# A chunked recurrence and two dense layers on one core: units of 64 tokens of all batches, and two tensor segments per chunk

## The chip, the cores and the metric

The kernel runs on one core of a Trainium2 chip. The metric is the device time of one execution in microseconds (us). Three executions of the kernel before took 1132.85, 1128.9 and 1137.99 us; the median is 1132.85 us. An "engine" here is TensorE (PE, matmuls), VectorE (DVE), ScalarE (ACT), GpSimd (POOL) or SyncE (SP, which issues most of the transfers).

## The reference

There are 4 batches, 8 heads, 768 tokens and a head size of 40. Each of the 32 sequences (batch, head) carries a 40 by 40 state through its tokens:

```python
for t in range(S):
    y[:, :, t] = np.einsum('bhd,bhde->bhe', rt, state)
    Sa = np.einsum('bhde,bhe->bhd', state, at)
    state_decay = state * wt[:, :, None, :] - np.einsum('bhd,bhe->bhde', Sa, bt)
    state = state_decay + np.einsum('bhd,bhe->bhde', vt, kt)
```

The output, as 3072 tokens by 320 features, goes through two layers. Layer 1 is `h = x @ w_in; x = max(0.01 h, h) @ w_out` with 2048 hidden features. Layer 2 is `sigmoid(x @ w_gate) * (x @ w_val) @ w_out` with 1536 hidden features. All of it is float32.

## The kernel before

**Recurrence.** The 768 tokens are cut into 6 blocks of 128 tokens and each block into 2 halves of 64 tokens. A *unit* u is 128 tokens (block u // 2) of half of the batches, so there are NU = 12 units. A unit has two *chunks* of 64 tokens, n = 2u and 2u + 1, so there are NT = 24 chunks. A chunk holds 16 sequences, as TQ = 8 pairs; the two sequences of a pair lie in partitions 0 to 63 and 64 to 127 (`half(0)`, `half(1)`). The second chunk of a unit needs the state that the first one leaves; the first chunk of a unit needs the state of the second chunk of unit u - 2.

Within a chunk the recurrence is turned into small matmuls. Each function named below issues 8 or 16 pairs of them; the profile records each float32 matmul twice, so 16 small matmuls are "x32":
- `pe_a_ka` (L630, L636) makes the scores of b and k with a, for unit g + 2 and unit g + 1. From the b scores ScalarE makes `p_sb` (`act_a`), SP writes it to DRAM and loads it back in another layout (`store_p`, `load_p_top`, `load_p_low`), and VectorE inverts a triangular matrix column by column (`inverse_columns`, L1252 and L1256, 31 columns per unit, each column waiting for the one before). `store_t` and `load_t` bring the inverse back as `t_sb`.
- `pe_rhs_begin`, `pe_rhs_end` (L658, L662) make the right-hand side from v and from the state. `pe_first` (L698) and `pe_cross` (L708) apply the inverse within the upper 32 tokens and carry it to the lower 32. `pe_ut_u` (L731, L734) makes u in both layouts.
- `pe_sn` (L719) transposes the state. `pe_st` (L748) makes the state's update, which VectorE adds and decays (`dve_st`). `pe_vrur` (L760, L762) makes the scores with r, which VectorE masks (`dve_vrur`, L1285). `pe_y_begin` (L774, state part) and `pe_y_end` (L783) make y. `pe_kb` (L649, L651) transposes k and b.

Between two such functions ScalarE or VectorE empties the PSUM bank. The recurrence uses banks 4 to 7. `claim`, `filled`, `emptied` and `multiplied` are waits on the bank's two counters `bank_filled` and `bank_emptied`.

**Layer 1** works on one block of 512 tokens (128 tokens of 4 batches) at a time, in 16 steps m per block: `up_products` (L808, 8 matmuls of 128x512 into bank 0), `act_g` and `dve_g_low` on the result (float32 values are split into a high part, `g_hi`, and a low part, `g_lo`, L1301), then `down_products` of the step before (L823 to L828, 8 matmuls into banks 1 to 3). Weights and x are split the same way. **Layer 2** follows (`gate_val_products` L858, `down2_products` L876 to L878).

**Order.** Every engine has its program written out in order; each waits for semaphores in that order. Before, the loop goes over windows g (one unit each) of 8 slots s. In each slot PE does one step m = 8g + s - LAG of layer 1 (LAG = 18, so that m = 0 falls in slot 2 of window 2) and one group of the recurrence: at s = 0 `rhs`, `sn`, `first`; at s = 1 `cross`, `a_ka`, `ut_u`; at s = 2 `st`, `vrur`; at s = 3 `rhs` of the second chunk woven with `y_begin` of the first, `y_end`, `first`; at s = 4 `cross`, `a_ka`, `ut_u`, `sn`; at s = 5 `st`, `vrur`; at s = 6 `y_begin`, `y_end`, between the up and the down products; at s = 7 `kb` of both chunks. Before m = 0 there is no layer 1 work; there `fill` (L894) issues matmuls of the identity that nobody reads, as a table says. The last 18 steps of layer 1 run without recurrence.

**Weights of layer 1** come in 8 pieces into a staging tile of 4 places (`load_piece` on POOL's queue); ScalarE writes the high parts (`split_hi`) and VectorE the low parts (`split_lo`) in windows 0 and 1.

## Time and profile before

| what | value |
|---|---|
| runs | 1128.9, 1132.85, 1137.99 us, median 1132.85 |
| profiled execution: its own time | the page gives none beside its span |
| profiled execution: span | 1129.2 us, 36605 instructions |
| first step of layer 1 starts | 158.38 us |
| first `gate_val_products` of layer 2 starts | 733.09 us |
| mean granted TensorE clock | 0.973 |

The profile is of one execution by the hardware profiler. "Busy" is the time in which an engine executed something; a wait is idle time. Small matmuls overlap each other, so the time of a group of them is read from the start of the group to the start of the next one. `PEclk` is the granted TensorE clock as a share of 2.4 GHz: 1.00 is 2.4 GHz and 0.50 is 1.2 GHz. The share of waits marked "issue" is time in which the engine waited for nothing that the profile shows.

### The profile page before, as it was taken

The page shows a single profiled execution, that of the slowest core. Times are in us where ns is not written, and L with a number is a line of the kernel's source. Part 1 is how long each engine was busy: PE and PEld are TensorE (multiplying, and loading weights), DVE is VectorE, ACT ScalarE, POOL GpSimd, SP SyncE. Part 2 cuts the span into 40 slices and gives each one's busy share as a digit, 9 for nine tenths or more (in the row PEclk, how much of TensorE's full clock was granted, in tenths as well). Part 3 has the DMA queues.
Part 4 walks back from the last instruction along what each step waited for, and adds up shares of the span by engine and source line. Part 5 has one row for each costly group of instructions (what it writes and reads, how often), then busy time and mean ns, then how long its engine had stood idle before and what let it go on. Part 6 is the DMA issues. An engine that isn't in the chain of part 4 may idle for free.

```text
span 1129.2 us, 36605 instructions
## 1 busy us (share of the span) xinstructions
PE 1072.3 (95%) x16106; PEld 917.0 (81%) x16106; DVE 595.8 (53%) x1306; ACT 397.3 (35%) x782; POOL 146.4 (13%) x179
## 2 busy tenths in 40 slices
PE   2888979999999999999999999999999999999998
PEld 2777868888888887788788788888888888888887
DVE  7797786767676776667574224443223232323222
ACT  2142243344444443533343335542222222222222
POOL 6313030403122121303010000000000000000000
PEclk9977679999999999999999999999999999999999
DMA  5836363344335342434333024220201002020000
GB/s 176 252 103 151 68 129 80 82 110 123 85 75 134 89 108 62 125 90 100 64 110 79 9 91 145 80 89 1 61 1 57 5 1 61 1 61 1 24 1 23
DMA packets 133856, 87.62 MB, mean 78 GB/s; under 512 B 98274, under 2 KB 113634, under 8 KB 133700
## 3 DMA queue, kind: packets, MB, share of 16 engines
q1 hardware_dynamic: 126740, 62.85, 22.8%
q0 software_dynamic: 6960, 22.45, 6.6%
q8 instruction: 127, 2.08, 0.8%
q14 instruction: 29, 0.24, 0.1%
HBM read 66.39 MB, written 18.87 MB: 76 GB/s over the span
## 4 chain that ended last, share of the span: by engine, by line
PE 89%; issue 4%; DVE 3%; ACT 1%; POOL 1%; DMA 0%; SPq 0%; ACTq 0%; POOLq 0%; DVEq 0%
PE bank L808 16%; PE bank L858 12%; PE pair L858 12%; PE bank L823 4%; PE bank L878 4%; PE bank L876 4%; PE bank L877 4%; PE bank L824 4%; PE bank L825 4%; PE bank L894 3%; PE bank L783 2%; PE bank L760 2%; PE bank L774 2%; PE bank L630 2%; PE bank L828 2%
## 5 line engine op out<-in xcount | busy, mean ns | idle before, releaser
L1301 DVE TENSOR_TENSOR g_lo<-g_full,g_hi 128x512 fp32r<-128x512 f32 x168 | 125.3, 746 | 229.8 <-ACT g_hi L1064 229.6
L1064 ACT CAST g_hi<-g_full 128x512 fp32r<-128x512 f32 x168 | 104.3, 621 | 134.7 <-DVE g_full L1354 131.6
L808 PE MATMUL bank<-x_hi,w_up 128*128 128x512 f32 x480 | 134.7, 410 | 3.6 <-issue 3.6
L1057 ACT ACTIVATE g_full<-bank 128x512 f32<-128x512 f32 x96 | 57.5, 599 | 210.0 <-PE bank L808 204.7
L1256 DVE TENSOR_TENSOR t_unit<-t_unit,prod 128x126 f32<-128x126 f32 (+22 forms) x372 | 106.5, 286 | 12.8
L1252 DVE TENSOR_TENSOR prod<-t_unit,p_unit 128x126 f32<-128x126 f32 (+22 forms) x372 | 102.1, 275 | 20.1 <-DMA p_unit<-p_dram 7.0
L808 PEld LDWEIGHTS bank<-x_hi,w_up 128*128 128x128 f32 x480 | 85.4, 189 | 23.0 <-issue 4.5
L1354 DVE TENSOR_TENSOR g_full<-pair,h_sb 128x512 f32<-128x512 f32 x36 | 24.9, 692 | 112.7 <-PE pair L858 112.0
L808 PE MATMUL bank<-x_lo,w_up 128*128 128x512 f32 x288 | 82.1, 393 | 0.0
L823 PE MATMUL bank<-g_hi,w_dn 128*128 128x512 f32 x192 | 76.4, 398 | 0.4 <-DVE g_lo L1301 0.2
L824 PE MATMUL bank<-g_hi,w_dn 128*128 128x512 f32 x192 | 75.0, 391 | 0.0
L1354 DVE TENSOR_TENSOR g_full<-bank,h_sb 128x512 f32<-128x512 f32 x36 | 24.9, 692 | 94.6 <-PE bank L858 86.3
L825 PE MATMUL bank<-g_lo,w_dn 128*128 128x512 f32 x192 | 74.8, 390 | 0.0
L808 PEld LDWEIGHTS bank<-x_lo,w_up 128*128 128x128 f32 x288 | 54.5, 189 | 12.2
L858 PE MATMUL pair<-x_hi,up 128*128 128x512 f32 x240 | 62.8, 391 | 0.0
L858 PE MATMUL bank<-x_hi,up 128*128 128x512 f32 x240 | 62.8, 391 | 0.0
L878 PE MATMUL bank<-dn,g_lo 128*128 128x320 f32 x192 | 59.3, 309 | 0.0
L877 PE MATMUL bank<-dn,g_hi 128*128 128x320 f32 x192 | 59.3, 309 | 0.0
L876 PE MATMUL bank<-dn,g_hi 128*128 128x320 f32 x192 | 59.1, 308 | 0.0
L630 PE MATMUL bank<-a_sb,b_sb 40*64 40x64 f32 x768 | 33.6, 248 | 23.0 <-POOL a_sb L301 21.6
L630 PEld LDWEIGHTS bank<-a_sb,b_sb 40*64 40x64 f32 x768 | 29.9, 159 | 25.7 <-issue 23.1
L858 PEld LDWEIGHTS bank<-x_hi,up 128*128 128x128 f32 x240 | 44.1, 188 | 7.9
(146 smaller groups left out, 2401.0 us busy)
## 6 DMA issues: line engine op xcount, KB each, us to landing
p_unit<-p_dram SPq DMA_DIRECT2D x48, 128.0 KB, 2.9
stage<-in_w_out POOLq DMA_DIRECT2D x7, 640.0 KB, 5.8
v_tok<-in_vT SPq DMA_DIRECT2D x12, 320.0 KB, 3.1
v_nu<-in_vN SPq DMA_DIRECT2D x24, 160.0 KB, 5.9
x<-y_sb SPq DMA_DIRECT2D x48, 80.0 KB
k_sb<-in_kF POOLq DMA_DIRECT2D x22, 160.0 KB, 3.4
v_sb<-in_vF SPq DMA_DIRECT2D x22, 160.0 KB
r_sb<-in_rF SPq DMA_DIRECT2D x22, 160.0 KB
```

Of the source, the lines that this page charges most:

```text
L808: last = nc.tensor.matmul(up_bank(m)[:], lhs, rhs, start=(e == 0), stop=(e == len(products) - 1))
L823: nc.tensor.matmul(bank[1 + kk][:], w_high, hi, start=(f == 0), stop=False)
L824: nc.tensor.matmul(bank[1 + kk][:], w_low, hi, start=False, stop=False)
L825: nc.tensor.matmul(bank[1 + kk][:], w_high, lo, start=False, stop=(f == NF1 - 1))
L858: last = nc.tensor.matmul(o[:], lhs, rhs, start=(x == 0), stop=(x == len(products) - 1))
L876: nc.tensor.matmul(o, g_hi[:, par, tok], wt[:, 0, f % GT], start=(f == 0), stop=False)
L877: nc.tensor.matmul(o, g_hi[:, par, tok], wt[:, 1, f % GT], start=False, stop=False)
L878: last = nc.tensor.matmul(o, g_lo[:, par, tok], wt[:, 0, f % GT], start=False, stop=(f == NF2 - 1))
L1064: nc.scalar.copy(g_hi[:, m % 2], g_full[:]).then_inc(g_hi_ready, 1)
L1252: nc.vector.tensor_tensor(terms, t_unit[:, 0:m, t:t + 1].to_broadcast([P, m, rest]), p_unit[:, t, t + 1:C].unsqueeze(1).to_broadcast([P, m ...
L1256: nc.vector.tensor_tensor(t_unit[:, 0:m, t + 1:C], t_unit[:, 0:m, t + 1:C], terms, ALU.add).then_inc(column_ready, 1)
L1301: nc.vector.tensor_tensor(g_lo[:, m % 2], g_full[:], g_hi[:, m % 2].bitcast(F32), ALU.subtract).then_inc(g_lo_ready, 1)
```

## The change

- **Units.** A unit is now 64 tokens of all batches; its two chunks are the two halves of the batches. Chunk n needs the state of chunk n - 2, no longer of chunk n - 1. The host lays the inputs out accordingly. Chunks 0 and 1 have no state, so their state matmuls are left out, and so are the state updates of the last two chunks.
- **Order.** The loop goes over chunks n with 4 slots each, m = 4n + s - 22. The recurrence has two segments per chunk: at s = 1 `rhs_begin(n)`, `sn(n-1)`, `vrur(n-1)`, `rhs_end(n)`, `st(n-1)`, `first(n)`; at s = 3 `cross(n)`, the scores (`a` of n + 4, `ka` of n + 1, woven with the state part of y of n - 1), `y_end(n-1)`, `ut_u(n)`, `kb(n+1)`. `fill` is gone.
- **Banks.** `st` and `y` go to bank 0, which they share with the up products; `ut` and `u` share banks 4 and 5; `sn` lies beside `rhs` in the same two banks.
- **Halves.** In every odd pair q the two sequences change places between partitions 0 to 63 and 64 to 127 in part of the operands (`side(i, q)`), also in v and r, which the host swaps.
- **Loads.** b, k, r and v are loaded per chunk instead of per unit; r and v have one place each instead of two. The vrur products have their own tile `vru`; the layer 1 output is evicted into `x_f`.
- **Weights.** Each layer 1 piece is loaded into its own final place and split there, with `x_f` as a scratch place for 64 rows; there is no staging tile. The splits move from before layer 1 to chunks 4 to 7, two pieces per chunk, at s = 2 and 3.

```diff
-LAG = 18
+LAG = 22
+        BANKS = dict(rhs=(4, 5), vrur=(6, 7), st=(0,), first=(6,), a=(6,), ka=(7,), y=(0,), utu=(4, 5), kb=(6, 7))
+        SLOT_X = [("rhs", 0), ("vrur", -1), ("st", -1), ("first", 0)]
+        SLOT_Y = [("a", 4), ("ka", 1), ("y", -1), ("utu", 0), ("kb", 1)]
...
@@ gpsimd_program
+            for n in range(-4, NT):
+                if n >= 0:
+                    fetch_k(pool, n + 2)
+                    fetch_b(pool, n + 4)
+                if chunk(n + 4):
+                    pool_a(pool, n + 4)
+                    pool_b(pool, n + 4)
+                if chunk(n + 2):
+                    pool_k(pool, n + 2)
+                if n >= 0:
+                    fetch_a(pool, n + 5)
+                if n == -1:
+                    pool.wait_ge(p_low_loaded, 32)
+                    load_piece(pool, 0)
+                    load_piece(pool, 1)
...
@@ sync_program
+            for n in range(NT + 2):
+                if n >= 2:
+                    store_y(sp, n - 2)
+                    load_v(sp, n - 1)
+                    load_r(sp, n - 1)
+                if n % 4 == 1 and n >= 5:
+                    load_x(sp, (n - 5) // 4)
+                if n >= 1:
+                    store_p(sp, n + 3)
+                if n % 2 == 0 and n >= 2:
+                    load_p_top(sp, (n + 2) // 2)
+                    load_p_low(sp, (n + 2) // 2)
+                load_w(sp, n + 5)
+                if n % 2 == 0 and n >= 2:
+                    load_v_nu(sp, n // 2)
+                if n % 2 == 1:
+                    load_v_tok(sp, (n + 1) // 2)
+                    store_t(sp, (n + 1) // 2)
+                    load_t(sp, (n + 1) // 2)
...
+        def side(i, q):
+            return i if q % 2 == 0 else 1 - i
...
@@ up_products
             wait(pe, g_ready, m if m <= DENSE else m - 1)
+            wait(pe, bank_emptied[0], turns_before_up[m])
...
-        FILL = {("kb", -1): 2, ("sn", 0): 56,
...
@@ tensor_program
+                    if s == 1:
+                        if chunk(n):
+                            pe_rhs_begin(pe, n)
+                        if has_state(n - 1):
+                            pe_sn(pe, n - 1)
+                        if chunk(n - 1):
+                            pe_vrur(pe, n - 1)
+                        if chunk(n):
+                            pe_rhs_end(pe, n)
+                        if has("st", n - 1):
+                            pe_st(pe, n - 1)
+                        if chunk(n):
+                            pe_first(pe, n)
+                    elif s == 3:
+                        if chunk(n):
+                            pe_cross(pe, n)
+                        pe_scores(pe, n + 4, n + 1, n - 1)
+                        if chunk(n - 1):
+                            pe_y_end(pe, n - 1)
+                        if chunk(n):
+                            pe_ut_u(pe, n)
+                        if chunk(n + 1):
+                            pe_kb(pe, n + 1)
...
@@ vector_program
                     if s == 1:
+                        if n % 4 == 1 and 5 <= n < 4 * NJ + 5:
+                            dve_x(dve, (n - 5) // 4)
+                        if chunk(n - 1):
+                            dve_vrur(dve, n - 1)
+                        if has("st", n - 1):
+                            dve_st(dve, n - 1)
+                    elif s == 3:
...
+                            if chunk(n + 1):
+                                dve_ka(dve, n + 1)
+                            if ahead:
+                                inverse_columns(dve, t, 10, 12)
+                            if chunk(n - 1):
+                                dve_y(dve, n - 1)
+                            if ahead:
+                                inverse_columns(dve, t, 12, 15)
```

The new `pe_scores` issues, for q in 0 to 3, first the y matmuls of pair 2q and the ka matmuls of pair q, then the a matmuls of pair q and the ka matmuls of pair q + 4, then the a matmuls of pair q + 4 and the y matmuls of pair 2q + 1.

## Rows read from the trace of the kernel before

**Rows 1.** The page, busy time of each engine and its share
```profile
PE 1072.3 (95%) x16106; PEld 917.0 (81%) x16106; DVE 595.8 (53%) x1306; ACT 397.3 (35%) x782; POOL 146.4 (13%) x179
```

**Rows 2.** The page, the chain that ended last, by engine
```profile
PE 89%; issue 4%; DVE 3%; ACT 1%; POOL 1%; DMA 0%; SPq 0%; ACTq 0%; POOLq 0%; DVEq 0%
```

**Rows 3.** Stretches: length, then busy PE, PEld, DVE, ACT, POOL; PEclk, DMA, GB/s
```profile
0.00:158.38 158.38, 118.07 (x2923) 108.55 (x2923) 125.25 (x303) 47.19 (x102) 53.30 (x66) 0.84 0.59 154
158.38:733.09 574.71, 562.75 (x11160) 464.35 (x11161) 353.14 (x835) 240.89 (x491) 92.61 (x112) 0.99 0.37 91
733.09:1129.20 396.11, 391.48 (x2025) 344.05 (x2023) 117.36 (x170) 109.21 (x190) 0.53 (x1) 1.00 0.09 28
...
300.88:353.21 52.33, 51.53 (x1153) 42.36 (x1152) 36.98 (x91) 20.57 (x45) 11.62 (x14) 1.00 0.38 88
```

**Rows 4.** Stretches of one unit, PE: kb; rhs, sn, first; and so on
```profile
300.88:302.89 2.01, 2.01 (x129) 1.00 0.27 94
...
306.75:308.00 1.25, 1.16 (x66) 1.00 0.52 151
308.00:308.90 0.90, 0.78 (x46) 1.00 0.08 18
308.90:309.59 0.69, 0.69 (x32) 1.00 0.00 0
313.99:314.69 0.70, 0.70 (x34) 1.00 0.65 129
314.69:315.67 0.98, 0.98 (x69) 1.00 0.73 142
315.67:316.71 1.04, 1.04 (x78) 1.00 0.65 156
320.60:321.34 0.74, 0.74 (x33) 1.00 0.60 205
321.34:322.43 1.09, 1.09 (x68) 1.00 0.55 85
326.31:328.24 1.93, 1.93 (x98) 1.00 0.00 0
...
335.49:336.99 1.50, 1.10 (x78) 1.00 0.04 11
336.99:337.73 0.74, 0.74 (x33) 1.00 0.00 0
...
345.46:346.48 1.02, 1.02 (x33) 1.00 0.24 38
346.48:347.51 1.03, 1.03 (x37) 1.00 0.95 152
```

**Rows 5.** Stretches: up products after small matmuls; ten dense steps of layer 1
```profile
302.89:304.84 1.95, 1.95 (x14) 1.61 (x9) 1.71 (x8) 0.76 (x2) 1.27 (x3) 1.00 0.11 23
...
695.01:731.28 36.27, 36.27 (x162) 30.04 (x160) 16.15 (x20) 18.84 (x27) 2.12 (x4) 1.00 0.29 102
```

**Rows 6.** Groups by line, page: the low part of g
```profile
L1301 DVE TENSOR_TENSOR g_lo<-g_full,g_hi 128x512 fp32r<-128x512 f32 x168 | 125.3, 746 | 229.8 <-ACT g_hi L1064 229.6
```

**Rows 7.** Groups by line, DVE, 0 to 158 us: columns and vrur masks
```profile
L1252 DVE TENSOR_TENSOR prod<-t_unit,p_unit 128x126 f32<-128x126 f32 (+22 forms) x106 | 31.7, 299 | 11.5 <-DMA p_unit<-p_dram 7.0 <-ACT t_unit L997 1.0
...
L1285 DVE TENSOR_TENSOR x_f<-bank,mask 128x512 f32<-128x512 f32 x8 | 5.1, 684 | 3.2 <-PE bank L762 3.2
```

**Rows 8.** DMA issues of 0 to 160 us: KB each, us to landing
```profile
t_dram<-t_unit SPq DMA_DIRECT2D x6, 128.0 KB, 4.1
...
x_f<-x SPq DMA_DIRECT2D x2, 128.0 KB, 7.1
```

**Rows 9.** Order in time: last column of unit 0, then its first use
```profile
44.16 0.18 DVE L1256 TENSOR_TENSOR t_unit<-t_unit,prod 128x16 f32<-128x16 f32 x1
...
55.40 0.76 PE L698 MATMUL bank<-rhs_sb,t_sb 32*32 32x40 f32 x32 [2.04 <-issue]
```

**Rows 10.** Stretch: the a and ka scores of one chunk at half clock
```profile
104.49:106.22 1.73, 1.73 (x65) 1.73 (x68) 1.66 (x3) 0.00 (x0) 1.73 (x4) 0.50 1.00 223
```

More of the change, by code:

```diff
@@ new lines, in pe_vrur @@
+        def pe_vrur(pe, n):
+            claim(pe, "vrur", n)
+            pe.wait_ge(v_loaded, 32 * (n + 1))
+            pe.wait_ge(r_loaded, 32 * (n + 1))
+            emptied(pe, "utu", n)
+            for q in range(TQ):
+                for j in range(2):
+                    nc.tensor.matmul(bank[6 + j][half(j), q * L:(q + 1) * L], v_sb[half(j, D), q],
+                                     r_sb[half(j, D), q], start=True, stop=True)
+                    last = nc.tensor.matmul(bank[6 + j][half(1 - j), q * L:(q + 1) * L], u_feat[half(j, D), q],
+                                            r_sb[half(j, D), q], start=True, stop=True)
+                    if q == TQ - 1:
+                        last.then_inc(bank_filled[6 + j], 1)
@@ L1054, in act_g @@
+            if not has("st", n):
+                last.then_inc(bank_emptied[4], 1)
         def act_g(act, m):
```

956 lines of the change are left out of this document (428 added, 528 removed).

## The prediction

> **What bounds the kernel now.** I read the page's busy times first: PE is busy 95% of the span, VectorE 53% [rows 1]. The chain of waits is PE for 89% of its time, and "issue" for 4% [rows 2]. Then stretches [rows 3]. Before the first layer 1 step (158.4 us) PE is busy 118.1 us, fill included, and VectorE 125.3: a latency-bound start. From there to layer 2, 574.7 us long, PE stands idle for only 574.7 - 562.8 = 12 us. Layer 2 (396 us) is dense, and no edit touches it except x_f as o's home, which the last dense block hides. So the kernel is PE work plus a start, and the sum has two terms.
>
> The profiled span is 1129.2 us, and the page gives no other time of that execution; the median of the runs is 3.65 above it. I sum against 1129.2 and add 3.65 at the end.
>
> **Term 1: from the first up products to layer 2 (574.7 us).** Ten dense steps take 36.27 us, so a step is 3.63 and 96 steps are 348.3 [rows 5]. One whole unit takes 52.33 [rows 3]. Its small groups are in [rows 4]; six more of its second chunk repeat rows within 0.01 (y_end 1.02, first 0.70, cross 0.69, a/ka 0.99, st 0.74, vrur 1.09). All twenty give 20.85. Eight dense steps are 29.0, so 52.33 - 20.85 - 29.0 = 2.5 us is lost where small and large matmuls meet, 0.31 for each of 8 insertions; the up products after small ones take 1.95 instead of 1.81 [rows 5]. One wait of the unit is in it, so I take 0.26.
>
> After the change a chunk costs, by the same rows:
> - Segment s = 1. Rhs is 32 + 32 records; the a/ka group shows 64 records in 0.98 [rows 4], and the other 0.27 of rhs's 1.25 is the wait on `rhs_begun`, now behind sn and vrur: 0.98. Sn uses two of the array's four quarters, 0.74; with alternate halves all four, as kb does at 2.01 / 128 = 15.7 ns a record, which would be 0.50. I take 0.55. Vrur 1.09, st 0.74, first 0.69 stay. Sum 4.05.
> - Segment s = 3. Cross 0.70. The state part of y alone is 1.02 for 32 records; woven into the scores it is 96 records at 0.98 / 64, 1.47 for all. Y_end 1.03, ut and u 1.07 (1.04 and 1.10 busy), kb half of 2.01. Sum 5.27.
>
> That is 9.32 per chunk, 18.6 per unit against 20.85. Sn's waits (rows of 0.90, and 0.40 idle in the 1.50) go; late next is first, which waits for rhs's copy behind st's 0.74.
>
> With LAG 22 the first up products follow segment 1 of chunk 5, so 18 segments of the first kind follow (72.9) and 19 of the second (100.1), then vrur and y of chunk 23 (3.1). Less 5.5 at the end: no a scores in four chunks (4 x 0.49), no st and u in two (2 x 1.2), no kb once (1.0). Sum 170.6. Insertions: 39 x 0.26 = 10.1.
>
> **Waits that the change adds**, none of which the trace shows as such:
> - Bank 0. Up products now wait until VectorE has emptied st or y. At s = 1, vrur ends 0.5 + 0.74 + 0.69 = 1.9 before the up products want the bank; VectorE needs two masks of 0.684 [rows 7] and an add of at most that: 1.9 to 2.05, a wait of about 0.15, 18 times, 3 us. At s = 3, ut/u and kb (2.1) cover one y of 0.7. Bounds 0 and, if five columns of 2 x 0.3 [rows 7] stand ahead each time, 3 us per segment.
> - Every fourth chunk `act_x` and `dve_x` (3 x 0.7) come before vrur's masks in VectorE's order: 1.4 us, 5 times, 7 us. Bounds 0 and 2.1 + 2 each, since x is stored, loaded and cast in 9.5 us after y.
> - Odd chunks: y, five columns of inverse and a decay now stand before g_low of s = 0: 0.25, ten times, 2.5 us.
> - Splits of the weights between steps: VectorE 3.5 us per chunk for four chunks, with its 37 of 49 us per unit already taken [rows 3]; 2.5 us (0 to 8). A piece is 2 or 3 ScalarE copies instead of one, and it has room (20.6 of 52.3 [rows 3]).
>
> Together 15 (0 to 40). POOL's queue issues 8 loads of b and k per unit instead of 4; it is busy 11.6 of 52.3 [rows 3], so that hides; SP has 4 more loads per unit, and r, now with one place, follows y's store. With 7.5 us of layer 1 between, that hides; at the start it doesn't. Of the 12 us idle I keep 7 (mostly "issue"), and add 3 for slow clock at the first steps.
>
> Term 1: 348.3 + 170.6 + 10.1 + 15 + 7 + 3 = 554.0, against 574.7: 20.7 less.
>
> **Term 2: the start.** The last column of unit 0 is done at 44.3 and used at 55.4 [rows 9]. These 11 us are t stored (4.1 to landing [rows 8]), loaded, with four weight pieces on the queues; two remain there, so I take 51. After that each unit is a chain on VectorE: in steady state 37.0 busy less eight g_low of 0.746 [rows 3, 6], 31 us per unit. The splits leave the start (8 pieces of 1.8, 14 us), a true gain. But r waits behind the round trip of t in SP's order (4.1, its issues, and a load), which stalls vrur by some 6 to 8: 38 per unit. Column runs end at 76 and 115, chunk 4's first runs at about 130; its segment 3 takes 12 at half clock. Then y is stored, x loaded (7.1 to landing [rows 8]) and cast before rhs's copy of chunk 5, since `act_x` stands first in ScalarE's order; up products at 155, against 158.4: 3.4 less, for one chunk more done. Bounds: 143 if r never stalls; 172 if units take the 47 us of before.
>
> The clock hangs on this. The a/ka scores take 1.73 at granted 0.50 (1.2 GHz), 0.98 at 1.00 [rows 10, 4], and PEclk is 0.84 in the start [rows 3] with fill running. Without fill PE has pauses, so I take 1.2 GHz for all of it: 2 x 9.32 x 1.75 = 33 us per unit, under VectorE's 38. By rows the start is not PE's. The Trainium skill (TensorE: Matmul & The Clock Gate, "Why this matters for your kernels") asks that TensorE stay busy without pauses, or the clock falls to half; that speaks against dropping fill. No row shows the start without fill. By that rule, if the doubled groups lay in the chain, the up products would come at 172.
>
> **Sum:** 1129.2 - 20.7 - 3.4 = 1105; plus 3.65, **1109 us**.
>
> **Rivals.**
> 1. *Bank 0 comes back late* (slower). VectorE is in order and at 75% in a unit; if columns stand before `dve_st` or `dve_y` when the bank fills, PE stands still at the up products. 24 us of gain over 38 segments is 0.63 each: more eats it, and 0.9 above the forecast's waits is slower by 1%. With 1.3 it is 1109 + 46 = 1155. For: st's slack is near zero. Against: VectorE waits 229.6 us for ScalarE before 168 g_low, 1.4 each [rows 6]: it is ahead, not behind. Chance 0.13.
> 2. *The start grows* through half clock and the r load: up products at 172, 1109 + 17 = 1126, no change by measure. For: three chains of like length (columns, POOL's b load, r) share it. Against: the splits' 14 us leave. Chance 0.15.
> 3. *The exchanged halves do nothing*: sn stays 0.74 and y's state part costs 0.53 more, 0.72 x 18.5 = 13: 1122. What speaks against is kb: it issues two matmuls of the same half in a row and still takes 15.7 ns a record, where y's state part takes 32 [rows 4]. So the use of all four quarters sets the pace. The Trainium skill (TensorE: Matmul & The Clock Gate, "Part 3: Packing small matmuls") says that a weight load overlaps running matmuls only when its row group differs; sn and y alternate row groups already, so by it alone this case would hold, and kb's row does not agree. Chance 0.07.
> 4. *More*: VectorE stays ahead (waits 5 instead of 15) and the start takes 143: 1109 - 22 = 1087. Chance 0.15.
> The forecast has 0.50, with its own range 1095 to 1121.
>
> **Numbers.** A measurement of this kernel can tell about 1% (11 us) from no change. Faster: forecast, case 4, half of case 3, 0.67. Same: case 2, the rest of 3 and the edges, 0.19. Slower 0.14. The range for 8 in 10 takes case 4 and case 2 and the upper bound of the waits: 1086 to 1138; beyond lie rival 1 and a little below.
>
> **What would show it.** A unit of two chunks in steady state should take 18.6 + 29.0 + 4 x 0.26 = 48.7 plus about 1 of waits, not 52.3; segments 4.1 and 5.3; scores of 96 records near 1.47, sn near 0.5. PE's waits before the up products should name VectorE's st (L1272's successor) for about 0.15 each. The up products should start at 155 and layer 2 at 709. PEclk in the first 155 us should be below 0.84. Wrong would be: a layer 2 start later than 725, waits of over 0.6 at the up products, or chunk 4's first later than 140.

## The result, and the profile after

The changed kernel takes 1179.99 us, the median of four runs (1178.18 to 1185.72), against 1132.28 for the kernel before on the same chip: ratio 1.0453, interval 1.0393 to 1.0514. It is 4.5% slower, where 1109 was forecast. Its profiled span is 1179.2 us.

Stretches of the changed kernel, columns as in [rows 3]: the start, layer 1 with the recurrence, layer 2.

```profile
0.00:169.32 169.32, 84.00 (x2625) 78.55 (x2625) 126.06 (x317) 40.93 (x94) 63.33 (x82) 0.77 0.55 145
169.32:783.11 613.79, 563.39 (x10876) 465.79 (x10873) 355.19 (x818) 248.60 (x481) 103.75 (x138) 0.95 0.33 84
783.11:1179.20 396.09, 391.47 (x2025) 344.05 (x2023) 117.36 (x170) 109.21 (x190) 0.53 (x1) 1.00 0.09 28
```

Against [rows 3] the start grew by 10.9 us, the second stretch by 39.1, layer 2 not at all. In the second stretch PE is busy as long as before (563.4 against 562.8) though it has fewer records to work on, and it stands idle for 50 us instead of 12. The granted clock there is 0.95, not 0.99. Both are the reader's first hint: work was saved, and the gain was lost again to waits and to half clock.

The page of the changed kernel: busy times, granted clock in 40 slices, and the chain that ended last.

```profile
PE 1038.9 (88%) x15520; PEld 888.4 (75%) x15520; DVE 598.6 (51%) x1303; ACT 398.7 (34%) x764; POOL 167.6 (14%) x221
...
PEclk9975669899999999989999999999999999999999
...
PE 71%; DVE 14%; DMA 4%; SPq 4%; issue 4%; ACT 1%; POOL 0%; DVEq 0%; ACTq 0%; POOLq 0%
```

Against [rows 1, 2] VectorE's share of the chain is 14%, from 3%, at the same busy time: its load is no bound, but it is late at places.

**The products of an undisturbed chunk came out near the forecast.** Groups of one chunk, columns as in [rows 3]; in order rhs's first half, sn, vrur, st, first, cross, scores with y's state part, y_end, ut/u, kb.

```profile
602.31:602.79 0.48, 0.48 (x33) 0.48 (x36) 0.27 (x1) 0.00 (x0) 0.00 (x0) 1.00 0.00 0
602.79:603.27 0.48, 0.48 (x48) 0.42 (x40) 0.00 (x0) 0.00 (x0) 0.00 (x0) 1.00 0.00 0
603.27:604.22 0.95, 0.95 (x68) 0.95 (x68) 0.00 (x0) 0.00 (x0) 0.00 (x0) 1.00 0.15 54
604.80:605.55 0.75, 0.75 (x40) 0.70 (x33) 0.75 (x2) 0.59 (x2) 0.00 (x0) 1.00 0.71 191
605.55:606.36 0.81, 0.76 (x37) 0.67 (x33) 0.78 (x3) 0.17 (x2) 0.00 (x0) 1.00 0.83 212
614.15:614.84 0.69, 0.69 (x33) 0.64 (x33) 0.27 (x1) 0.00 (x0) 0.00 (x0) 1.00 0.00 0
614.84:616.38 1.54, 1.54 (x69) 1.46 (x65) 0.33 (x1) 0.43 (x1) 0.00 (x0) 1.00 0.00 0
616.38:617.40 1.02, 1.02 (x36) 0.94 (x32) 0.95 (x4) 0.00 (x0) 0.00 (x0) 1.00 0.05 16
617.40:618.32 0.92, 0.92 (x69) 0.92 (x65) 0.89 (x3) 0.00 (x0) 0.00 (x0) 1.00 0.00 0
645.19:646.30 1.11, 1.11 (x72) 1.06 (x65) 0.00 (x0) 0.96 (x2) 0.00 (x0) 1.00 0.00 0
```

Sn takes 0.48 (0.55 forecast), scores with y's state part 1.54 (1.47), vrur 0.95 (1.09), first 0.81 (0.69), kb 1.11 (1.0). Sn and the woven scores, the two products that the exchanged halves were to shorten, are about as short as forecast. Over all chunks the list is too low; point 1 of the account below has the numbers.

I divided the second stretch of both kernels by walking its PE records: a group lasts from its start to the start of the next, less any wait of 0.15 us or more before that one; an up or down group of over 2.45 us is counted as 1.85 and the rest as half clock.

| us | before | after | forecast |
|---|---|---|---|
| up and down products at full clock | 366.5 | 359.7 | 358.4 |
| small products | 196.8 | 187.2 | 170.6 |
| waits and pauses | 9.5 | 45.9 | 22 |
| half clock in up and down products | 1.8 | 21.1 | 3 |
| sum | 574.7 | 613.9 | 554.0 |

Pauses inside a group stay in the group's time by this walk. With them PE's waits of 0.15 us or more are 49.9 us in all, 30.9 with a releaser named and 19.0 with none ("issue"); before they were 9.9, 3.8 and 6.0. Of the 16.6 us by which small products miss, 4.0 are such pauses and 4.3 are half clock, by the granted clock over their records. The rest are groups that take longer than the price list says.

What PE waits for in the second stretch: line and releaser, us in total, times, longest.

```profile
PE bank L884 <- DVE g_lo L1292: 15.6, 8, 5.3
PE bank L775 <- DVE vru L1278: 5.8, 4, 2.5
PE bank L828 <- DMA r_sb<-in_rF: 4.0, 4, 1.3
PE bank L817 <- issue: 3.6, 3, 1.4
PE bank L706 <- issue: 3.5, 4, 1.2
...
PE bank L869 <- DVE y_sb L1286: 1.2, 2, 0.9
...
PE bank L869 <- DVE st_sum L1268: 0.6, 2, 0.3
```

Three things stand there. The down products (L884) wait for g's low part. Pauses "issue", for nothing that the profile's waits show, of 0.4 us and more are 22 with 18.2 us, before 7 with 5.7. The waits for bank 0 (y_sb, st_sum), on which I had put most thought, are under 2 us.

### The profile page after: what moved, and what is told of

It reads as the page before. It is cut to its first block, busy times and chain, and to the rows that moved or that the text cites. A ratio compares the mean times of both kernels' runs of the same rounds, so it can differ in the third digit from the quotient of the medians.

```text
span 1179.2 us, 35633 instructions
## 1 busy us (share of the span) xinstructions
PE 1038.9 (88%) x15520; PEld 888.4 (75%) x15520; DVE 598.6 (51%) x1303; ACT 398.7 (34%) x764; POOL 167.6 (14%) x221
## 3 DMA queue, kind: packets, MB, share of 16 engines
q8 instruction: 123, 2.02, 0.7%
## 4 chain that ended last, share of the span: by engine, by line
PE 71%; DVE 14%; DMA 4%; SPq 4%; issue 4%; ACT 1%; POOL 0%; DVEq 0%; ACTq 0%; POOLq 0%
PE bank L869 12%; PE bank L919 11%; PE pair L919 11%; DVE prod L1250 4%; DVE t_unit L1254 4%; PE bank L939 4%; PE bank L937 4%; PE bank L938 4%; PE bank L884 3%; PE bank L885 3%; PE bank L886 3%; PE bank L842 2%; PE bank L889 1%; PE bank L888 1%; PE bank L775 1%
## 5 line engine op out<-in xcount | busy, mean ns | idle before, releaser
L869 PE MATMUL bank<-x_hi,w_up 128*128 128x512 f32 x480 | 138.2, 420 | 6.2 <-ACT x_hi L1083 2.3
L1250 DVE TENSOR_TENSOR prod<-t_unit,p_unit 128x126 f32<-128x126 f32 (+22 forms) x372 | 110.9, 298 | 22.6 <-DMA p_unit<-p_dram 8.5
L869 PEld LDWEIGHTS bank<-x_hi,w_up 128*128 128x128 f32 x480 | 91.6, 198 | 27.6 <-issue 3.6
L1254 DVE TENSOR_TENSOR t_unit<-t_unit,prod 128x126 f32<-128x126 f32 (+22 forms) x372 | 105.6, 284 | 12.8
L884 PE MATMUL bank<-g_hi,w_dn 128*128 128x512 f32 x192 | 79.1, 412 | 15.7 <-DVE g_lo L1292 15.6
L869 PE MATMUL bank<-x_lo,w_up 128*128 128x512 f32 x288 | 86.7, 412 | 0.0
L885 PE MATMUL bank<-g_hi,w_dn 128*128 128x512 f32 x192 | 77.0, 401 | 0.0
L446 POOL DMA_DIRECT2D k_sb<-in_kF x44 | 22.6, 517 | 342.4 <-PE bank L708 342.4
L869 PEld LDWEIGHTS bank<-x_lo,w_up 128*128 128x128 f32 x288 | 57.9, 201 | 13.1
L884 PEld LDWEIGHTS bank<-g_hi,w_dn 128*128 128x128 f32 x192 | 37.9, 197 | 29.7 <-DVE g_lo L1292 19.4
L828 PE MATMUL bank<-r_sb,v_sb 40*64 40x64 f32 x768 | 32.4, 243 | 30.3 <-DMA r_sb<-in_rF 29.0
```

What stands on the lines that cost most here:

```text
L869: last = nc.tensor.matmul(up_bank(m)[:], lhs, rhs, start=(e == 0), stop=(e == len(products) - 1))
L884: nc.tensor.matmul(bank[1 + kk][:], w_high, hi, start=(f == 0), stop=False)
L885: nc.tensor.matmul(bank[1 + kk][:], w_low, hi, start=False, stop=False)
L1250: nc.vector.tensor_tensor(terms, t_unit[:, 0:m, t:t + 1].to_broadcast([P, m, rest]), p_unit[:, t, t + 1:C].unsqueeze(1).to_broadcast([P, m ...
L1254: nc.vector.tensor_tensor(t_unit[:, 0:m, t + 1:C], t_unit[:, 0:m, t + 1:C], terms, ALU.add).then_inc(column_ready, 1)
```

## Why g_lo is late

VectorE at the longest of these waits (PE stands from 220.9 to 226.26): start, duration, engine, line.

```profile
216.33 0.30 DVE L1254 TENSOR_TENSOR t_unit<-t_unit,prod 128x136 f32<-128x136 f32 x1
217.33 0.43 DVE L1323 TENSOR_TENSOR w_dn<-dn_raw,w_dn 128x256 fp32r<-128x256 f32 x1 [0.70 <-ACT w_dn L1120]
217.68 1.22 DVE L1325 TENSOR_TENSOR w_dn<-dn_raw,w_dn 128x1024 fp32r<-128x1024 f32 x1
218.95 1.24 DVE L1226 TENSOR_TENSOR_SCAN decay<-w_raw,restart 128x520 f32<-128x520 f32 x1
220.47 2.15 DVE L1235 TENSOR_TENSOR_SCAN inv<-w_raw,restart 128x520 f32<-128x520 f32 x1
222.83 1.25 DVE L1254 TENSOR_TENSOR t_unit<-t_unit,prod 128x128 f32<-128x128 f32 x1
224.18 1.09 DVE L1250 TENSOR_TENSOR prod<-t_unit,p_unit 128x135 f32<-128x135 f32 x1
225.52 0.68 DVE L1292 TENSOR_TENSOR g_lo<-g_full,g_hi 128x512 fp32r<-128x512 f32 x1
```

Columns, a weight split, the decay and two more columns lie in order ahead of g_lo, and three of these operations are stretched: the scan that makes `inv` takes 2.15 where its mean in the start is 1.39, and column operations of 0.30 take 1.25 and 1.09. POOL multiplies in those moments (its `a_sb` from 220.34 to 221.52, `b_sb` from 222.76 to 223.93, `k_sb` from 223.89 to 225.12). The kernel before has such operations too, 20 column operations of over 0.6 us against 28 here, so the stretching alone does not make the waits; no run takes POOL's products away.

## The experiments

All ratios are against the kernel before on the same chip. "Start" is the time to the first up products; "layer 1" is from there to layer 2. The changed kernel is 1.0453, start 169.3, layer 1 613.8, PE waits and pauses in layer 1 45.9, slow up products (over 2.6 us) 9. All columns but the ratio are read from one profiled execution. Executions of one kernel lie up to 15 us apart (e13: 1152.84 to 1167.91), so a few us between two rows say little.

| run | ratio (interval) | start | layer 1 | waits | slow ups |
|---|---|---|---|---|---|
| e1 fill | 1.0557 (1.0503 to 1.0611) | 178.4 | 612.5 | 50.6 | 7 |
| e2 early splits | 1.0338 (1.0281 to 1.0395) | 181.3 | 588.4 | 37.4 | 6 |
| e3 VectorE's order | 1.0282 (1.021 to 1.0354) | 169.1 | 594.3 | 39.4 | 6 |
| e4 r early | 1.0446 (1.0398 to 1.0494) | 168.2 | 612.2 | 48.7 | 8 |
| e5 before without fill | 0.9954 (0.993 to 0.9979) | 155.7 | 576.1 | 13.0 | 1 |
| e7 x later | 1.0472 (1.043 to 1.0514) | 171.7 | 618.4 | 57.4 | 4 |
| e8 r from ScalarE | 1.0465 (1.0405 to 1.0526) | 171.0 | 623.7 | 49.1 | 11 |
| e9 four groups | 1.0536 (1.0483 to 1.0588) | 165.9 | 635 | 69.1 | 11 |
| e10 own banks | 1.0455 (1.0407 to 1.0503) | 169.6 | 606.7 | 35.9 | 6 |
| e11 and order | 1.0472 (1.0424 to 1.052) | 171.0 | 619.1 | 41.8 | 6 |
| e12 and all | 1.0665 (1.061 to 1.072) | 177.4 | 631.5 | 49.4 | 6 |
| e13 order, spread splits | 1.0271 (1.0208 to 1.0335) | 168.3 | 595.2 | 37.3 | 8 |
| e14 four tuned | 1.0317 (1.0261 to 1.0373) | 170.2 | 594.5 | 36.7 | 7 |
| e15 the same, LAG 22 | 1.0241 (1.0183 to 1.0298) | 161.7 | 593.4 | 36.5 | 7 |
| e16 light columns | 1.0229 (1.0161 to 1.0297) | 156.9 | 590.2 | 34.8 | 5 |
| e17 four, columns spilled | 0.9981 (0.9951 to 1.0011) | 159.4 | 569.3 | 19.2 | 5 |
| e18 four, SP's queue | 0.9919 (0.9887 to 0.9951) | 161.1 | 564.5 | 13.7 | 3 |

**e1: idle matmuls back in the start.**

```diff
+        FILL = {('kb', -1): 2, ('first', 0): 2, ('cross', 0): 2, ('kb', 0): 6, ('sn', 1): 4, ('st', 1): 12, ...
...
+                nc.tensor.matmul(bank[1][:, 0:P], ident[:], ident[:], start=True, stop=True)
...
```


> The changed kernel with idle matmuls (identity times identity into bank 1, which nothing uses before the first down products) back in the start, 28 before the first exclusive product, and 4 to 36 before the vrur and first groups of chunks 0 to 4, where TensorE stands still for 4 to 7.7 us now. Theory A (the start is held by the clock: vrur 1.98, st 1.30, first 1.28, scores and y at 1.2 GHz, about twice their full-speed times): granted clock of the first 169 us rises to over 0.8, each chunk's chain of products falls by up to 5 us, up products at 150 to 158 instead of 169.3, whole kernel 1160 to 1168. Theory B (the start is held by r's load and by VectorE's columns, TensorE waits for them): the clock rises, but the waits for r grow by as much as the products shrink, up products at 166 to 172, 1175 to 1183.

The clock of the start rose from 0.77 to 0.90 and the start got 9 us longer: 1190.35. VectorE's wait for the vrur products grew from 18.2 to 23.8. Theory A falls, and the time lies beyond Theory B's range too: raising the clock with fill does not buy the start back. What the same products would take at full clock without fill in PE's order, this run does not show. **e5** asks the same of the kernel before:

> The kernel before with all its idle matmuls of the start left out (266 of them, 45.9 us of TensorE in the first 158 us); the work is otherwise the same. Theory A (fill is worth little here, as bringing it back into the changed kernel gave nothing: the start is held by VectorE and by round trips): layer 1 starts at 156 to 162 instead of 158.4, the whole within 4 us of before. Theory B (without fill the doubled small groups come into the chain): the granted clock of the start falls from 0.84 to about 0.65, layer 1 starts at 165 to 172, whole kernel 1135 to 1142.

Leaving out all fill made the kernel before 0.5% faster (1127.93), its start 2.7 us shorter, with the start's clock at 0.78 instead of 0.84. That is Theory A and a little more.

**e2: the weight splits in chunks 0 to 3.**

```diff
-                    if 4 <= n < 8 and s >= 2:
-                        split_lo(dve, 2 * (n - 4) + s - 2)
+                    if 0 <= n < 4 and s >= 2:
+                        split_lo(dve, 2 * n + s - 2)
...
```


> The changed kernel with the eight splits of layer 1's weights in chunks 0 to 3, ahead of the up products, instead of 4 to 7 between them. Theory A (a split of 1.6 to 1.9 us on VectorE ahead of g_lo holds up the down products, and what follows a wait runs at half clock): the four g_lo waits of 2.73, 5.35, 2.77 and 1.17 at 194 to 286 us go, the granted clock of 169 to 287 rises from about 0.92 to 0.98, and that stretch gets 15 to 20 us shorter; the start grows by 5 to 14 because eight splits now stand in VectorE's chain there; whole kernel 1165 to 1177. Theory B (the clock between 169 and 287 is low for another reason, the transition from the start): the stretch gains only the waits, 8 to 12, and the start loses as much: 1178 to 1185.

g_lo waits fell from 15.6 to 3.3 and layer 1 by 25.4, more than the waits; the start took 12 back. At 1166.16 this is Theory A.

**e3: only VectorE's order** (columns 0 to 17 in even chunks, 18 to 21 behind g_lo (`dve_g_low`) of s = 0, none ahead of g_lo and the masks at s = 1).

```diff
-                        if behind:
-                            inverse_columns(dve, t, 15, 17)
-                    elif s == 1 and behind:
-                        inverse_columns(dve, t, 17, 22)
...
+                    if s == 0 and behind:
+                        inverse_columns(dve, t, 18, 22)
...
```


> The changed kernel with only VectorE's order changed: 18 instead of 15 columns of the inverse in even chunks, where VectorE waits 2.5 to 4.5 us for ScalarE before each g_lo, none between decay and g_lo of s = 0 nor ahead of g_lo and vrur's masks at s = 1 in odd chunks. Theory A (VectorE's order makes the waits, 15.6 us for g_lo and 5.8 for vrur's masks from 169 us on, and each longer one brings a run at half clock): of these 21.4 us half to two thirds go and of nine slow up products five go, 20 to 30 us in all, 1150 to 1160. Theory B (these waits are made by the splits and by x, whatever the columns do): up to 8 us less, 1172 to 1180.

Layer 1 is 19.5 shorter, 1159.64. Of 21.4 us of waits for VectorE 7 went and slow up products fell from 9 to 6. The time is inside Theory A, but fewer waits and slow products went than it said. **e13** spreads the splits as well:

> The changed kernel (two groups per chunk, bank 0 shared) with VectorE's order and the spread splits alone. Theory A (the waits for g_lo, 10.2 us with the order alone, are the splits standing behind y and ahead of the decay): they fall to 2 to 3, and half clock behind them; 8 to 15 us less than the order alone (1159.6), 1145 to 1152. Theory B (they come from elsewhere): no more than 4 less. The pauses behind long runs of small matmuls stay in both, 14 to 18 us.

g_lo waits fell from 10.3 to 5.8 but the total did not move (1159.59), which is Theory B's time: "issue" pauses and r's waits stood in their place, and there were eight slow up products.

**e4: r and v ahead of y's store and of t's load.**

```diff
+                if n % 2 == 1 and n >= 2:
+                    load_v(sp, n - 1)
+                    load_r(sp, n - 1)
                 if n >= 2:
                     store_y(sp, n - 2)
-                    load_v(sp, n - 1)
-                    load_r(sp, n - 1)
...
                     store_t(sp, (n + 1) // 2)
+                    load_v(sp, n)
+                    load_r(sp, n)
                     load_t(sp, (n + 1) // 2)
```


> The changed kernel with only SP's queue reordered: v and r of the next chunk are loaded ahead of the store of y, and at odd chunks between the store of t and its load, instead of behind both. Theory A (r's load behind t's round trip holds the start: 25 us of waits for r between 50 and 170 us): waits for r in the start fall to 5 to 10, up products at 152 to 160, from 169.3; the four waits for r of 0.8 to 1.3 us later go too; whole kernel 1163 to 1172. Theory B (VectorE's columns and t are as long as r, so another wait takes over, first on t or on vrur's masks): up products at 164 to 170, 1173 to 1180.

SP's queue in the changed kernel, after the last column of unit 1 (vrur waits for r until 92.12):

```profile
80.42 1.27 SPq L521 DMA_DIRECT2D t_dram<-t_unit  x2
84.24 1.92 SPq L532 DMA_DIRECT2D t_sb<-t_dram  x4
86.22 0.85 SPq L541 DMA_DIRECT2D x<-y_sb  x2
87.19 1.01 SPq L462 DMA_DIRECT2D v_sb<-in_vF  x2
88.63 0.66 SPq L470 DMA_DIRECT2D r_sb<-in_rF  x2
```

PE's waits in the start of the changed kernel (44 to 169.32), and then in e4 (44 to 168.19):

```profile
PE bank L828 <- DMA r_sb<-in_rF: 25.0, 4, 7.5
...
PE bank L775 <- DVE vru L1278: 9.3, 3, 4.2
```
```profile
PE bank L778 <- DVE vru L1281: 19.0, 3, 10.0
PE bank L831 <- DMA r_sb<-in_rF: 5.8, 2, 3.3
```

r's wait went as meant, 25.0 to 5.8, and the start kept 168.2: the masks are late now, and VectorE waits 10.9 us for the rows of p, which SP loads later. Theory B. **e8** sends r and v through ScalarE's queue (`load_r(act, n)` behind `act_kb`) instead:

> The changed kernel with v and r of each chunk loaded from ScalarE's queue, right behind its copies of kb, so that they stand neither behind y's store nor behind t's round trip, and SP's queue has only the rest. Theory A (one queue in order is what holds the start: r in the changed kernel, the rows of p when r was put ahead of them): waits for r under 5 us in the start and none for p, up products at 155 to 162 instead of 169.3, whole 1166 to 1174. Theory B (the start's length is VectorE's work and the product chain): another wait takes the time, up products at 166 to 170, whole 1176 to 1182. The four issues per chunk cost ScalarE under 1 us, which has room.

The waits for r stayed 19.3 of 25.0 and nothing was won (1185.61, beyond both ranges). Why r is still late there is open.

**e7: x one step later.**

```diff
-LAG = 22
+LAG = 23
...
```


> The changed kernel with layer 1 one step later against the chunks (LAG 23 instead of 22): x is cast and split at s = 2, after vrur's masks and the state, and used at s = 3. Theory A (x_lo ahead of vrur's masks, 3 x 0.69 us on VectorE, makes the wait of first in every fourth chunk, and the half clock behind it): the waits of first for the masks, 5.8 us from 169 us on, fall under 1.5, the wait for x_hi of 2.3 at 723 goes, 3 or 4 of the nine slow up products go; the start grows by 0 to 4: in all 1164 to 1174. Theory B (x is late by its own load, store of y to landing of x 10.5 us): no gain from the order, a wait for x in its place, 1177 to 1184.

Waits for the masks fell from 5.8 to 1.6 and x's wait at 723 us went as Theory A said, and slow up products fell to 4. But the up products wait 1.4 to 2.1 us at six places with "issue" as releaser, and the down products 2.3 for o's eviction. At 1186.72 it is beyond both ranges: moving x moved the wait.

**e9: four groups per chunk**, so that a layer 1 step lies between any two (with e4's queue).

```diff
-        SLOT_X = [("rhs", 0), ("vrur", -1), ("st", -1), ("first", 0)]
-        SLOT_Y = [("a", 4), ("ka", 1), ("y", -1), ("utu", 0), ("kb", 1)]
+        SLOTS = [[("utu", -1), ("kb", 0)], [("rhs", 0), ("vrur", -1)],
+                 [("st", -1), ("first", 0)], [("a", 4), ("ka", 1), ("y", -1)]]
...
```


> The changed kernel with its small products in four groups per chunk instead of two: ut/u and kb at s = 0, rhs, sn and vrur at s = 1, st and first at s = 2, the rest at s = 3 (and SP's order with r ahead of t's load, which alone changed nothing, 1178). Theory A (TensorE's pauses with nothing waited for come behind a run of more than about 150 small matmuls: 21 of over 0.4 us, 17.7 us in the changed kernel with 246 on average between layer 1 steps, 7 of 5.7 us before with 129): they fall to 5 to 8, with them most of the nine slow up products; the wait of first for vrur's masks goes, since a step lies between; against it stand 36 more insertions of 0.26, 9.4 us: 1155 to 1166. Theory B (the pauses have nothing to do with the length of a run of small matmuls): they stay at 15 to 20 and the insertions come on top, 1180 to 1190.

PE's waits in its layer 1:

```profile
PE bank L872 <- DVE st_sum L1275: 33.1, 12, 5.9
PE bank L872 <- issue: 21.4, 5, 10.8
PE bank L872 <- DVE y_sb L1293: 20.2, 20, 1.4
```

The 10.8 of the second line is the wait ahead of the very first up products and belongs to the start. The mechanism of Theory A is confirmed and its time is not (1195.0, beyond both ranges). Pauses of 0.4 us or more inside runs of small matmuls went from 21 to 2, with about 120 records between steps instead of 240. But now the up products (L872) stand at bank 0, which st and y share: here st, first and the up products follow each other directly. One of these waits shows why it is so long:

```profile
444.82 0.19 DVE L1257 TENSOR_TENSOR prod<-t_unit,p_unit 128x31 f32<-128x31 f32 x1 [6.69 <-DMA p_unit<-p_dram]
...
447.77 0.48 DVE L1275 TENSOR_TENSOR st_sum<-bank,st_sb 128x320 f32<-128x320 f32 x1
```

VectorE stood for p's rows, which SP had not loaded since it was waiting with t's load, and st's bank lay behind that in VectorE's order.

**e10 to e12** move st out of bank 0 into bank 7, which it shares with vrur, ka and kb, and put y's last products ahead of other work.

```diff
-        BANKS = dict(rhs=(4, 5), vrur=(6, 7), st=(0,), first=(6,), a=(6,), ka=(7,), y=(0,), utu=(4, 5), kb=(6, 7))
+        BANKS = dict(rhs=(4, 5), vrur=(6, 7), st=(7,), first=(6,), a=(6,), ka=(7,), y=(0,), utu=(4, 5), kb=(6, 7))
...
```


> The kernel with four groups per chunk (1195), and two edits against its waits of the up products for bank 0, 52 us in all: the state goes into bank 7 instead of bank 0, and y's last products stand before the second half of a's scores and the cross products, about 0.95 us of work behind which VectorE empties bank 0. Theory A (the shared bank 0 is the bound of that kernel: the up products stand at a bank that VectorE has not read): the waits for st_sum go, those for y_sb fall under 0.4 each, the 11 slow up products fall to 3 or 4; 70 to 80 us less in layer 1, whole kernel 1115 to 1130. Theory B (VectorE is late by itself and somebody else waits in place of the bank): g_lo or the rhs begin waits instead, 1150 to 1175.

The waits for st_sum went and y_sb's fell from 20.2 to 8.6: 1179.89, 15 us better than e9, not 70, and short of both theories. A mistake of mine is in it: with the order of the scores changed, they and y's state part take 1.78 + 0.61 us per chunk instead of 1.54, 45.6 us in all instead of 30.3. The half of y's state part that was woven with a's scores now stood beside ka's.

> The same, with VectorE's order of the run that gave 1159.6 (more columns in even chunks, none ahead of g_lo at s = 0 and 1 in odd ones). Theory A (that order is right whatever the groups): the waits for g_lo behind the splits and the decay fall, 5 to 15 us less than the run without it. Theory B (with a layer 1 step between all groups VectorE has slack everywhere): within 3 us of it.

No better, as Theory B said, but not for its reason: g_lo waits 20.4 instead of 9.1. The order of VectorE that helped with two groups did not help with four. **e12** added x later and the spread splits:

> The same with x cast and split at s = 2 and used at s = 3 (LAG 23), and the weight splits spread: four in chunks 3 and 4, one each at s = 0 and 1 of chunks 6 and 8, where VectorE stands idle. Theory A (what is left of the waits between 169 and 290 us is the splits, and at each block x): waits in layer 1 fall under 15 us in all, 10 us less than the run before; layer 2 starts at about 710 to 715, whole kernel 1105 to 1118. Theory B (the step later and the earlier splits cost the start what they save): the same as the run before within 4 us.

1204.08, the worst: x's casts stood behind first's copy on ScalarE, and the up products waited 3.0 at four blocks; start 177.4.

**e16: VectorE's column operations cut to one element** (the inverse is not computed; count and order stay).

```diff
-                m, rest = t // 2 + 1, C - 1 - t
+                m, rest = 1, 1
...
```


> The changed kernel with each of the inverse's column operations cut to one element per partition (same count, order and waits; the inverse is not computed, so this leaves out most of VectorE's 17 us of column work per unit). Theory A (VectorE late is the larger part): the waits for g_lo and vrur's masks, 21.4 us in layer 1, fall under 6, half-clock runs with them, layer 1 gets 25 to 35 us shorter; the start gets 10 to 20 shorter: 1130 to 1145. Theory B (the pauses inside the runs of small matmuls and x are the larger part): pauses stay at 15 to 20 us and the slow up products at 6 or more, layer 1 gains 10 to 18; the start, held by r's round trip, gains under 6: 1155 to 1168.

1151.62, between the two. The profiled execution was the fastest of its four (1144.94), so the stretches show some 7 us too much gain. The start is 12.4 shorter though r's waits stay at 17.4: most of these 12 us are the columns'. Layer 1 is 23.6 shorter. The g_lo waits of 2.73, 4.84 and 2.79 at the splits stay, so those are the splits' and the decay's, not the columns'; the later ones go, but one of 0.7. Pauses go on, 17 with 12.8 us.

**e14 and e15: four groups with everything placed by the traces so far**: e9's groups, st in bank 7, cross behind y_end, the scores woven as in the changed kernel, VectorE's columns laid where it waits for ScalarE, p's store ahead of t's load. In e14 x is used a step later (LAG 23), in e15 it is not.

```diff
+                at = (0, 5, 10, 12, 15, 17, 22, 27) if t <= 3 else (0, 4, 9, 10, 10, 18, 22, 26)
...
+        DVE_SPLITS = {(4, 2): [0], (4, 3): [1], (6, 0): [2, 3], (6, 1): [4, 5], (8, 0): [6, 7]}
```


> Four groups per chunk, the state in bank 7, y's last products ahead of the cross products, the scores woven as in the changed kernel (the run with own banks spent 45.6 us on scores and y's state part instead of 30.3), VectorE's columns laid where it waits for ScalarE (none between y and g_lo of s = 0), splits at s = 0 and 1 of chunks 6 and 8, x at s = 2 and used at s = 3, and p's store ahead of the wait for t. Theory A (nothing else bounds it): small products 185 us, up and down products 366, idle under 18, half clock under 8: layer 1 577, start 170, whole 1135 to 1146 with idle as said. Theory B (with a step between all groups VectorE still falls behind in each unit, 37 of 52 us busy plus POOL's stretching): g_lo waits of 15 to 20 stay, 1155 to 1170.

> The same with x used at s = 2 (LAG 22). Theory A (x is late there by its store, load and cast: 3.4 us at three blocks, each with a slow up product behind it): start 2 to 4 us shorter, layer 1 15 us longer, 10 us more than with LAG 23. Theory B (x's casts at s = 2 stand ahead of first's copy and cost as much): the same within 4.

g_lo waits are gone in both. What is left is mostly x at four or five blocks, 2.3 to 5.5 us each, nearly always with a slow up product behind it. The time of e14 is Theory B's, its waits are not. In e14, 1162.94, x's low part ended at 280.84 and the up products began at 280.94: VectorE had columns, masks, g_lo and st ahead of it. e15 (1153.67) is 9 us faster, all of it start, against both its theories: x a step later made the start 8.5 us longer, more than the step of 3.6, and layer 1 no shorter.

**e17** starts from e14 and changes the order at these places: on VectorE x's low part right behind the masks and the last four columns in the next unit's first slot, on ScalarE x ahead of the rhs copy and o's eviction ahead of a's, and t's transfers on SP with the columns.

```diff
+                    if s == 0 and n % 2 == 0 and 8 <= n < NT:
+                        inverse_columns(dve, n // 2, 27, C - 1)
...
```


> The kernel with four groups and x used at s = 3, with x's low part at s = 1 right behind vrur's masks, the last four columns of each inverse moved into the next unit's first slot (VectorE idles there), none ahead of the masks at s = 1, o's eviction ahead of a's, and in the start the masks ahead of five columns. Theory A (VectorE's order is what is left): the waits of the up products at blocks fall from 4.1 to under 1, those for o's eviction (1.2, three times) go, the slow up products fall from 7 to 2 or 3; layer 1 570 to 575 long instead of 594.6; the start 4 to 8 shorter: whole kernel 1128 to 1140, level with the kernel before. Theory B (other waits, for t or p, take the place, since each column run now ends later): 1150 to 1165.

1126.91, level with before and a little under Theory A's range; layer 1 is 25 us shorter than in e14. **e18** moves o's store behind t's load and r ahead of t's store, and starts the spill of columns a unit earlier:

> As e17, with o's store (3.1 us of issues in SP's queue, ahead of the rows of p and of t) behind t's load, r's and v's loads ahead of t's store in the start, and the spill of the last columns from the fourth unit on. Theory A (SP's order and these columns are what the waits are): the two waits of first of 2.5 us and their slow up products go (8 us), the waits for r in the start fall from 9.4 to under 4, layer 1 starts at 153 to 157: 1112 to 1120, faster than both kernels. Theory B (o's store or t takes the place): 1123 to 1130.

1119.55, faster than before by 0.8% (0.9919, 0.9887 to 0.9951), the best of all. The interval lies below 1, but the difference is of the size that the prediction called too small to tell. Its stretches:

```profile
0.00:161.13 161.13, 87.54 (x2624) 81.26 (x2625) 118.72 (x307) 41.13 (x94) 63.40 (x82) 0.79 0.58 152
161.13:725.66 564.53, 549.38 (x10875) 450.96 (x10873) 349.55 (x828) 247.11 (x481) 101.80 (x138) 0.98 0.35 91
```

The products and VectorE's work are those of the changed kernel. The groups (four), st's bank and the order on every engine are not, and layer 1 is 49 us shorter. The whole lies in Theory A's range, the start does not (161.1): PE no longer waits for r there, but 8.1 us for the masks.

## Why the prediction was wrong, point by point

The span is 74.2 us over the forecast of 1105: small products 16.6, waits and pauses 23.9, half clock 18.1, up and down products 1.3, the start 14.3. The step that failed is the price of PE's idle time and of the half clock behind it. The sum gave it 15 + 7 + 3 = 25 us, and the second stretch shows 45.9 + 21.1 = 67. Rival 1 had a slower kernel in it (0.13), but by bank 0, and that was not the cause.

1. **Products: right in kind, too cheap in all.** Up and down products with their insertions came out at 359.7 (358.4 forecast). In the chunk shown the groups are within 0.15 us of the list. Over all chunks, waits taken out, rhs takes 1.18 a chunk instead of 0.98, kb 1.17 instead of 1.0, first 0.86 instead of 0.69, vrur 0.99 instead of 1.09. Small products were to fall by 26 us (196.8 to 170.6) and fell by 9.6, or 13.6 without the pauses inside them; in e18 by 18.5. Rival 3 (exchanged halves do nothing) is out, since sn fell from 0.74 to 0.48 and the scores with y's state part take 1.54. The halves were not tried apart from the rest. In e18 the second stretch is 10.2 us shorter than before, where 20.7 was forecast.
2. **"Waits that the change adds ... 15 (0 to 40)": mis-sized, and its parts wrong.** Waits with a releaser named are 30.9 us, 27 more than before: inside the range, at twice the value. Splits were given 2.5 us; with y, the decay and columns they made waits of 2.73, 5.35 and 2.77 (e2, e16). I had read VectorE's 37 of 49 us as room. Its work is in order, and what counts is the longest run of it between two g_lo. The mean of 1.4 us that VectorE waits before g_lo [rows 6] said the same and hid the same: of the 76 g_lo beside the recurrence in the kernel before, 28 found VectorE without 0.15 us of it. Bank 0, given 3, cost 1.8 in the changed kernel; it became rival 1's mechanism only in e9.
3. **"Of the 12 us idle I keep 7 (mostly "issue")": mis-sized.** "Issue" is 19.0 us, 18.2 of it in pauses of 0.4 and more. The pauses come with long runs of small matmuls, and two segments per chunk make these about 240 records instead of about 125. Run e9 shows it, and the last section says what PE waits for there.
4. **"Add 3 for slow clock": mis-sized most**, 21.1 in up and down products, and 4.3 in small ones. I took half clock as a matter of the start. The last section has the rows.
5. **Start 155: wrong, 169.3; rival 2's size (172), not its reason.** The unit period was 42 to 45, not 38. VectorE was busy 126.1 in the longer start, not 14 less than before [rows 3]: two of the eight splits still lie there (3.6 us, from 14.2), and one more chunk brings 6 us of columns, 3 of scans and 1 of masks. VectorE's idle time grew by 10, and its wait for the vrur products alone from 3.2 to 18.2. Of the loop of three (columns, p, r), r alone gives nothing: e4 took 19 us of r's waits away and gained 1.1. The columns do: e16 gained 12.4 with r's wait in place. More clock by fill did not help (e1, e5). What holds the rest of the start is open.

The conclusion is that the idea saved products, though half of what was forecast (seven tenths in e18), and that the order written around it gave back more. That two groups per chunk are a loss by themselves is not shown: no kernel with two groups and all of e18's order was run.

## What to carry to other kernels

Where a step is nearly all TensorE, price the waits by the longest run of in-order work between two results that TensorE wants, not by the other engine's share of busy time. Count what a wait costs with the half clock that can come behind it. Take the pieces of such a change one by one to the trace: removing one wait moved it to another place four times (e4, e7, e9, e13). Runs e2 and e3 won back 14 and 20 us of 48, and only placing all together came below the kernel before.

## What the runs showed of the hardware that I had not expected

**A short pause can cost more than itself.** The changed kernel at a pause of 1.61 us: PE's records, and then the stretches, whose seventh figure is the granted clock.

```profile
377.08 0.33 PE L775 MATMUL bank<-rhs_sb,t_sb 32*32 32x40 f32 x6
379.02 1.09 PE L775 MATMUL bank<-rhs_sb,t_sb 32*32 32x40 f32 x26 [1.61 <-issue]
380.03 2.50 PE L869 MATMUL bank<-x_hi,w_up 128*128 128x512 f32 x5
```
```profile
377.08:380.03 2.95, 1.34 (x36) 1.12 (x32) 2.68 (x11) 0.17 (x1) 0.92 (x2) 0.80 0.63 170
380.03:383.61 3.58, 3.58 (x10) 2.81 (x9) 0.52 (x3) 0.43 (x1) 0.00 (x0) 0.50 0.34 96
383.61:386.42 2.81, 2.81 (x9) 2.21 (x8) 1.22 (x4) 1.22 (x2) 0.00 (x0) 0.64 0.00 0
```

The up products run at 0.50 (1.2 GHz) and take 3.58 instead of 1.95, the down products 2.81 instead of 1.9: 2.5 us lost behind 1.6. The kernel before had no such stretch in layer 1 behind its first step; its pauses were 1.25 us at most. Not every pause does this: over all nineteen traces up products were slow behind 46 of 49 pauses of over 2.2 us, behind 22 of 59 of 1.25 to 2.2, behind 12 of 205 of 0.5 to 1.25, and 18 times of 1484 with none of 0.5 close ahead. The Trainium skill (TensorE: Matmul & The Clock Gate, "Why this matters for your kernels") asks that TensorE be kept busy, without idle gaps between its matmuls; by this trace that is right in layer 1. In the start it was worth nothing: there the clock rose from 0.77 to 0.90 and the time with it (e1).

**Long runs of small matmuls wait for their own instructions.** Of the changed kernel's 22 pauses of 0.4 us or more with no releaser, 20 lie behind at least 150 records of small matmuls. All kernels with two groups per chunk have 16 to 25 such pauses inside their small matmuls, those with four groups 1 to 6, the kernel before 4. The page of the changed kernel names a queue of the kind "instruction": 123 packets of 16 KB, 2.02 MB.

```profile
q8 instruction: 123, 2.02, 0.7%
```

In all nineteen traces together, 220 of the 223 such pauses ended 1.15 to 1.65 us after one of these packets had landed. By chance it would be 7 or 8 in a hundred, and of the 252 waits with a releaser named it was 23. The packet of the pause above landed at 377.65, and PE went on at 379.02. A packet comes for about 250 records of PE and PEld together (87 packets in layer 1), and in no trace did two land less than 3.2 us apart there. By an estimate from these numbers a segment of 240 records of small matmuls, with as many of weight loads, wants two packets in its 4.1 to 5.3 us and can outrun them, and half of it cannot. No run changed the loading itself.

**VectorE is held while POOL multiplies.** VectorE and then POOL in the changed kernel:

```profile
403.90 0.29 DVE L1250 TENSOR_TENSOR prod<-t_unit,p_unit 128x121 f32<-128x121 f32 x1
404.22 1.15 DVE L1254 TENSOR_TENSOR t_unit<-t_unit,prod 128x121 f32<-128x121 f32 x1
405.40 1.14 DVE L1250 TENSOR_TENSOR prod<-t_unit,p_unit 128x110 f32<-128x110 f32 x1
406.57 0.27 DVE L1254 TENSOR_TENSOR t_unit<-t_unit,prod 128x110 f32<-128x110 f32 x1
...
403.93 1.29 POOL L327 TENSOR_TENSOR b_sb<-b_sb,inv 128x512 f32<-128x512 f32 x1 [3.71 <-DMA b_sb<-in_bF]
405.18 1.23 POOL L336 TENSOR_TENSOR k_sb<-k_sb,inv 128x512 f32<-128x512 f32 x1
```

Of 744 column operations in the changed kernel the 25 that began during one of POOL's products took 1.16 us (median), the others 0.26; POOL has three such products per chunk, in the kernel before too. VectorE's masks, one input of which lies in PSUM, are not held: in e18 28 of them began during a POOL product and took 0.68 (median), like the rest. The Trainium skill (VectorE: DVE Perf Modes, "Two Vector instructions with no wait between them") mentions that the second SBUF read of a two-input instruction is shared with GpSimd; these rows agree.
